# Attention stage of a fused attention and two-MoE kernel: 1/Q by one 128x512 reciprocal per unit instead of two two-column reciprocals and two backward scans

## The reference

```python
state = 0                                   # (B, H, D, D)
for t in range(S):
    cur = einsum('bhd,bhe->bhde', u * k[t], v[t])
    y[t] = einsum('bhd,bhde->bhe', r[t], state + cur)
    state = w[t][..., None] * state + einsum('bhd,bhe->bhde', k[t], v[t])
x = y as (3072 tokens, 384)
x = moe1(x)   # top-1 of 8 experts, 384 -> 1024 -> 384, relu, scaled by the gate
x = moe2(x)   # the same with a sigmoid output gate
```

## Time and profile before

| | |
|---|---|
| median of 3 runs | 793.58 us |
| lowest, highest | 788.15 us, 794.45 us |
| the profiled execution | 787.61 us, span 785.9 us, mean granted TensorE clock 0.979 |
| PE busy | 726.7 us (92% of the span) |
| DVE busy | 502.6 us (64%) |
| ACT busy | 389.8 us (50%) |
| POOL busy | 159.8 us (20%) |

### The profile page before, as it was taken

The page is one execution under the profiler, slowest core; times in us unless marked ns, Lnnn a source line. Parts: engine busy times, 40 slices in busy tenths (PEclk is TensorE's granted clock), DMA queues, the critical chain, the costliest instruction groups (busy, mean ns, idle before and its releaser), DMA issues.

```text
span 785.9 us, 20353 instructions
## 1 busy us (share of the span) xinstructions
PE 726.7 (92%) x5566; PEld 646.2 (82%) x5567; DVE 502.6 (64%) x1359; ACT 389.8 (50%) x761; POOL 159.8 (20%) x202
## 2 busy tenths in 40 slices
PE   2998898983999999999999998799999999999993
PEld 2787777763899999999999997699999999999993
DVE  7999999996567665847667674464444445336521
ACT  3666777781546454536456463154343535245421
POOL 5445566553000000000000001000111000000000
PEclk9999999996999999999999999899999999999998
DMA  6666688625735251505253351353333333316110
GB/s 135 155 156 157 183 261 244 161 95 176 271 106 168 94 170 40 192 28 172 85 169 119 120 184 37 119 195 108 133 110 120 124 125 113 120 35 196 40 35 27
DMA packets 50268, 103.75 MB, mean 132 GB/s; under 512 B 7921, under 2 KB 29904, under 8 KB 50224
## 3 DMA queue, kind: packets, MB, share of 16 engines
q1 hardware_dynamic: 29536, 67.18, 27.1%
q10 hardware_dynamic: 15568, 21.76, 10.3%
q0 software_dynamic: 5120, 14.26, 5.0%
HBM read 85.73 MB, written 19.01 MB: 133 GB/s over the span
## 4 chain that ended last, share of the span: by engine, by line
PE 76%; DVE 13%; issue 5%; DMA 2%; POOL 1%; ACT 1%; DVEq 0%; POOLq 0%; SPq 0%; ACTq 0%
PE bank L1320 20%; PE bank L1346 20%; PE bank L1354 10%; PE bank L1325 10%; PE bank L1335 6%; DVE SF L773 3%; DVE Q L764 3%; PE bank L1309 2%; PE bank L1287 2%; DVE Kb L778 1%; PE bank L1280 1%; DVE dv L783 1%; DVE YT L816 1%; PE bank L1136 1%; PE bank L1201 1%
## 5 line engine op out<-in xcount | busy, mean ns | idle before, releaser
L1320 PE MATMUL bank<-wall,xT_hi 128*128 (+1 forms) x660 | 180.0, 408 | 1.3 <-ACT xT_hi L655 1.3
L1346 PE MATMUL bank<-wall,hT_hi 128*128 x880 | 164.9, 338 | 0.5 <-ACT hT_hi L664 0.5
L1346 PEld LDWEIGHTS bank<-wall,hT_hi 128*128 128x128 f32 x880 | 153.0, 188 | 3.1 <-issue 0.7
L1320 PEld LDWEIGHTS bank<-wall,xT_hi 128*128 128x128 f32 x660 | 119.1, 191 | 22.0 <-issue 1.8
L879 DVE TENSOR_TENSOR wall<-raw,wall 128x1024 f32 (+1 forms) x96 | 112.0, 1221 | 31.3 <-ACT wall L561 28.2
L659 ACT ACTIVATE hs<-bank 128x512 f32<-128x512 f32 x110 | 65.3, 594 | 129.6 <-PE bank L1325 129.6
L1038 DVE TENSOR_TENSOR xT_lo<-bank,xT_hi 128x384 fp32r<-128x384 f32 x57 | 31.8, 558 | 107.4 <-ACT xT_hi L655 107.4
L561 ACT ACTIVATE wall<-raw 128x1024 f32 (+1 forms) x96 | 95.0, 1051 | 10.4 <-issue 10.4
L1325 PE MATMUL bank<-wall,xT_lo 128*128 (+1 forms) x330 | 94.9, 396 | 0.0
L664 ACT ACTIVATE hT_hi<-bank 128x512 fp32r<-128x512 f32 x110 | 59.9, 596 | 68.6 <-PE bank L1335 68.6
L1354 PE MATMUL bank<-wall,hT_lo 128*128 x440 | 91.2, 349 | 0.0
(11 more groups left out here) (196 smaller groups left out, 983.4 us busy)
## 6 DMA issues: line engine op xcount, KB each, us to landing
raw<-wall_in SPq DMA_DIRECT2D x96, 512.0 KB, 3.8
xin<-sorted ACTq DMA_DIRECT2D x59, 194.0 KB
rk<-rk_in SPq DMA_DIRECT2D x46, 192.0 KB
v_in<-v_src ACTq DMA_DIRECT2D x24, 192.0 KB
vT<-vT_in ACTq DMA_DIRECT2D x48, 96.0 KB
wb<-w_in SPq DMA_DIRECT2D x46, 96.0 KB
sorted<-padrow SPq DMA_DIRECT2D x16, 194.0 KB, 2.0
sorted<-yrow,slot POOLq DMA_INDIRECT x28, 2.6
```

Source lines behind the costliest of these rows:

```text
L1320: pe.matmul(bank[n][:, :], xT_hi[:, k, :], w[:, bass.ds(slot, 1), cols].rearrange("p o n -> p (o n)"), start=(k == 0 and w is w_hi), stop= ...
L1346: pe.matmul(bank[2][:, 0:DM], hT_hi[:, j, :], w[:, bass.ds(slot, 1), W2 + j * DM:W2 + (j + 1) * DM].rearrange("p o n -> p (o n)"), start=( ...
```

## The change

Q is inverted directly: one reciprocal reads the 128 products of each of the four pairs and writes 128x512 values into `SF`, which loses its spare columns. The two reciprocals of two columns, the two backward scans and the four waits behind them go. The wait for `SF` (`sf_ready`) moves from in front of `route` and `Rq` to in front of `Kb`, so `Rq` now stands directly behind the reciprocal (behind `route`, where there is one). `wb` loses two constant columns per buffer, and `bank7` is cleared over 258 columns and no longer over 512.

```diff
-LASTQ = C1 + 2
-            wb = sb1("wb", [P, 2, SEG + 2])
+            wb = sb1("wb", [P, 2, SEG])
-            SF = sb1("SF", [P, SEG])
+            SF = sb1("SF", [P, PAIRS, C])
                 v.memset(rk[:, i], 0.0).then_inc(dve_const, 1)
-                link(v.memset(wb[:, i, SEG:], 0.0))
 
             clear(0)
-            link(v.memset(bank[7][:, :], 0.0))
+            link(v.memset(bank[7][:, 0:HSEG], 0.0))
                 v.wait_ge(q_ready, 2 * u + 2)
 
                 whole = Q[:, kq].rearrange("p (a t) -> p a t", t=C1)
-                for hf in range(2):
-                    v.reciprocal(bank[7][:, LASTQ + C - 1:LASTQ + HSEG - 1:C1], whole[:, 2 * hf:2 * hf + 2, C]).then_inc(iq_ready, 1)
-                    v.wait_ge(iq_ready, 2 * u + hf + 1)
-                    top = (hf + 1) * HSEG - 2
-                    v.tensor_tensor_scan(SF[:, top:(None if hf == 0 else HSEG - 1):-1], wb[:, par, top + 2:hf * HSEG + 1:-1],
-                                         bank[7][:, LASTQ + HSEG - 2:LASTQ - 1:-1], 1.0, ALU.mult, ALU.add).then_inc(sf_ready, 1)
-                    v.wait_ge(sf_ready, 2 * u + hf + 1)
+                v.reciprocal(SF[:, :, :], whole[:, :, 1:C1]).then_inc(sf_ready, 1)
                 route()
                 v.tensor_tensor(Rq[:, k], rk[:, par, 0], whole[:, :, 0:C], ALU.mult).then_inc(r_ready, 1)
-                v.tensor_tensor(Kb[:, k], rk[:, par, 1], SF.rearrange("p (a t) -> p a t", t=C1)[:, :, 0:C], ALU.mult).then_inc(k_ready, 1)
+                v.wait_ge(sf_ready, u + 1)
+                v.tensor_tensor(Kb[:, k], rk[:, par, 1], SF[:, :, :], ALU.mult).then_inc(k_ready, 1)
```

More of the change, by code:

```diff
@@ L196, in build @@
         pad0_done = [sem(f"pad0_done{m}") for m in range(2)]
-        q_ready, iq_ready, sf_ready, r_ready, k_ready = (sem(n) for n in ("q_ready", "iq_ready", "sf_ready", "r_ready", "k_ready"))
+        q_ready, sf_ready, r_ready, k_ready = (sem(n) for n in ("q_ready", "sf_ready", "r_ready", "k_ready"))
         wchk_step, w_checked, sq_done = sem("wchk_step"), sem("w_checked"), sem("sq_done")
```

## The result

The changed kernel takes 817.08 us (median of 5, 815.32 to 817.47) beside 793.58 us (median of 5, 788.15 to 795.01). The ratio is 1.0307, with a 95% interval of 1.0276 to 1.0338: slower by 23.5 us, forecast were 30. The profiled execution took 817.08 us, with a span of 815.3.

A forecast was written before the change was run, and what follows sets the result against it. DVE's instruction stream was taken to bound the attention, whose end shifts the whole. 24 x (3.35 - 0.09 - 1.87) = 33.4, less 3.5 for masking, gives +29.9 on the median 793.6: 824 us, range 798 to 858.

The forecast's parts named there:

- What bounds the stage: Attention, 8.6 to 166.8 us: DVE's instruction stream bounds it, busy 96%; `pre` of all 24 units lies on it.
- a floor some 11 us below: Attention, 20 to 160 us: PE has only 11.0 us idle, so it takes over beyond that gain.
- R: Length of the new 512-column reciprocal in each unit: 3.35 us, break-even at 1.96 us.
- The reading that hit: Four divisions against a one-column tensor-scalar: 6.2 ns per column, 3.35 us for the new reciprocal; forecast chance 0.34.
- The other readings: New reciprocal's length: streaming 0.68 us (chance 0.14), one-to-four-column slope 2.38 (0.26), one-to-two-column step 4.76 (0.22).
- The block: DVE's inversion before `Rq`, 24 units: 1.87 us goes, 3.35 less 0.09 comes, 33.4 us more in the sum.
- Masking: `Rq` and `Kb` later in the unit, clear of POOL's masking: 0.145 us per unit, 3.5 us taken back.
- POOL locked out: Rival: reciprocal takes both ports, POOL's masking waits, DVE loses 0.4 us per unit; +10 us, 834 us, chance 0.04.
- Profile and median: Final sum: profiled execution 6.0 us under the runs' median; +29.9 us put on 793.6 instead, giving 824, not 817.5.
- PE's waits: Attention: PE waits for `Kb` in nearly all units, some 1.4 us longer each.
- The granted clock: PE's clock stays at 1.0; a fall within the attention from long gaps was named as an unpriced risk.

The follow-up runs named there:

- Experiments 2 and 5: 2: kernel before, two of four pairs by one 128x256 reciprocal, 802.15 us; 5: changed kernel, copy replacing the reciprocal, table written 11.1 us before that of before.
- the regrouped scans: Kernel before with both forward scans, both short reciprocals, `Rq`, both backward scans, then `Kb`, second pattern in SBUF: 789.31 us, ratio 0.9970.

## Why the prediction was right

The direction, the mechanism and the range were right; the sum was 6.4 us too high.
- **What bounds the stage: right.** DVE's stream with nothing waiting inside it, `pre` of all 24 units on it, and a floor some 11 us below. Experiments 2 and 5 show the slope and the floor (14.3 us for half, -11.1 us for a copy). That PE alone is the floor did not hold: the loads of r and k have a larger share in DVE's waits.
- **R: right.** 3.35 us forecast, 3.353 measured. The reading that hit took four divisions against the fixed cost of an operation without one. It hit partly by luck: the four-column row lies on the line 153 + 6.25 n, but that of one column lies 6 ns above it, and so does that of two columns, by 8 ns, with PSUM's share in it. The other readings failed as the text had feared, by differences of some ns between widths where the steps are uneven, and by the target in PSUM. The Trainium skill's repeat count of 8 ("VectorE: DVE Perf Modes", Walkthrough), read as eight cycles per column, would have given 4.4 us; the run shows six cycles at the 0.96 GHz of that page.
- **The block: right.** 24 x (3.27 - 1.87) = 33.6 us, the same in all 24 units, forecast 33.4. The next instruction started 0.08 us ahead of the reciprocal's end.
- **Masking: right in kind.** Taken back were 24 x (0.105 + 0.075) = 4.3 us, forecast 3.5; the surplus is `Rq` itself, which shows 0.63 us behind a reciprocal that it need not wait for. With 0.2 us at the start and 0.3 of a wait this makes the 28.8 us of the first table.
- **POOL locked out: refuted.** The masking runs inside the reciprocal at its usual length.
- **Profile and median: the step that failed.** "The difference doesn't hang on it, and I put it on the median" took the profiled execution's lead of 6.0 us for an offset that both kernels share. It was not. Against its own profile the forecast was 817.5, and 817.08 was measured; put on the median it became 824. The profiled execution was the fastest of before that the record has. The two others profiled contain 3.1 and 4.5 us more up to the first table (in the second mostly DVE's waits), and 2 to 3 us more behind it (600.0 and 600.8 us; 597.8 in the first profile, 598.5 in the changed kernel). That the longer units of the changed kernel cover such waits fits its profile, which has none, but no experiment shows it, and why it is shorter behind the table than a usual execution of before stays open.
- **PE's waits: half right.** They were to come in nearly all units, and came 13 times from 30 to 195 us (13.8 us).
- **The granted clock: wrong.** It fell to 0.50 in places within the attention, where the text expected 1.0. DVE did not wait for PE there, so no time hung on it.

## What to carry to other kernels

Count a DVE reciprocal at 6.25 ns per column, six times what a tensor-scalar into PSUM adds ((695 - 228) / 448 = 1.04 ns); over 512 columns, with the fixed parts, it is 4.8 times. A scan with fewer divisions (690 ns for 257 columns, 2.7 ns each) is cheaper even with two short reciprocals and four waits around it. A price per column that comes out of rows of one to four columns can be off by a third to a half (4.3 and 9 for 6.25 here): bound it from several rows, and take the one that compares with the same operation's fixed part. And where the engine that bounds a stage leads the next one by only a few per cent, look for waits before you count a gain in full: the regrouped scans saved 6.6 us and then waited 6.0 for PE. Executions of one kernel can differ by such waits too, so look at the spread of the runs before adding a sum to the median.

## What was not expected of the hardware

- The reciprocal scales with 6.25 ns per column from 8 columns to 512, whether into SBUF or PSUM, while tensor-scalar into SBUF takes about six tenths of its PSUM time (426 to 695 ns at 512 columns).
- It doesn't disturb POOL, nor POOL it: 24 reciprocals took 3352 to 3355 ns beside masking, products and DMA issues on POOL. An operation with two SBUF inputs does meet the masking: means of 680 to 895 ns for the same 128x512, by where it lies. So does a copy from SBUF to SBUF: 427 ns at the shortest, 0.90 us where it ran beside the masking.
- A wait of 3.0 us on PE was followed by the lower clock, and 16 matmuls took 2.08 us instead of 1.16.
- A wait of DVE for its own last instruction costs 0.12 us: behind the reciprocal the next one started 0.08 us ahead of its end without a wait, 0.04 us after it with one, in all 24 units.
